# First batch of a two-scale attention kernel: q, k of later pairs loaded ahead of v, two q sums on POOL, and the last pair's transposes copied by two engines

## The reference

```
q_d, k_d, v_d = mean over each 4 positions of q, k, v          # 144 positions
out_up    = repeat(softmax(q_d k_d^T / 8) v_d, 4)              # coarse, full attention
out_local = softmax(q k^T / 8 where |i - j| < 4) v             # fine, a band
x = (out_up + out_local) laid out as 2304 tokens x 512
x = leaky_relu(x w_in1, 0.01) w_out1
h = x w_in2;  out = (h - tanh(h)) w_out2
```

## Time and profile before

| | |
|---|---|
| median of three runs | 960.9 us |
| the profiled execution | 960.35 us, of which span 958.6 us |
| PE busy | 942.1 us (98%) |
| PE weight loads busy | 884.8 us (92%) |
| DVE / ACT / POOL busy | 547.4 / 559.8 / 403.8 us |
| chain that ended last | PE 82%, POOL 6%, ACT 4%, issue 3%, DVE 2%, DMA 2% |
| granted clock in 40 slices | 8 tenths in the first slice, 9 or more tenths in every other |
| first slice (24 us) | PE 7 tenths busy, DVE 6, ACT 4, POOL 3, DMA 6 |

### The profile page before, as it was taken

How to read it: one execution, slowest core, us unless ns; L and a number is a source line. 1 busy time by engine, 2 the same in 40 slices (tenths; PEclk the granted TensorE clock), 3 DMA queues, 4 the chain that set the end, 5 groups by cost and what they waited for, 6 DMA issues and landing times.

```text
span 958.6 us, 19883 instructions
## 1 busy us (share of the span) xinstructions
PE 942.1 (98%) x6996; PEld 884.8 (92%) x6996; DVE 547.4 (57%) x1098; ACT 559.8 (58%) x1355; POOL 403.8 (42%) x343
## 2 busy tenths in 40 slices
PE   7999999999999999999999999999999999999998
PEld 6789999999999999999999999899899898898997
DVE  6754355435634543553235576776676766766764
ACT  4765546446445455454455677675666666656754
POOL 3584616427236246163342757433233232333232
PEclk8999999999999999999999999999999999999999
DMA  6875112211221121112002112000000000000000
GB/s 141 199 203 140 27 28 50 51 26 25 50 48 26 27 50 26 26 27 67 1 1 93 52 56 82 12 29 1 34 0 0 33 0 0 33 0 0 34 1 33
DMA packets 87797, 41.48 MB, mean 43 GB/s; under 512 B 60352, under 2 KB 81344, under 8 KB 87744
## 3 DMA queue, kind: packets, MB, share of 16 engines
q1 hardware_dynamic: 87744, 40.78, 16.3%
HBM read 36.04 MB, written 4.72 MB: 43 GB/s over the span
## 4 chain that ended last, share of the span: by engine, by line
PE 82%; POOL 6%; ACT 4%; issue 3%; DVE 2%; DMA 2%; SPq 1%; POOLq 0%; ACTq 0%; DVEq 0%
PE ph L520 13%; PE ph L521 12%; PE ph L522 12%; PE acc L596 6%; PE acc L549 6%; PE acc L597 6%; PE acc L598 6%; PE acc L550 6%; PE acc L551 6%; PE banks L418 2%; PE banks L450 2%; PE banks L437 2%; POOL g_lo L1135 1%; POOL in_lo L1114 1%; POOL w_lo_b L1142 1%
## 5 line engine op out<-in xcount | busy, mean ns | idle before, releaser
L1135 POOL TENSOR_TENSOR g_lo<-scratch,g_hi 128x384 fp32r<-128x384 f32 x96 | 126.1, 1313 | 257.1 <-ACT g_hi L723 257.1
L983 DVE TENSOR_TENSOR ph<-g,ph 128x288 f32<-128x288 f32 x128 | 59.0, 461 | 162.2 <-ACT g L737 161.7
L520 PE MATMUL ph<-x_hi,w_hi_a 128*128 128x288 f32 (+1 forms) x448 | 143.5, 320 | 0.8 <-DVE xT L873 0.5
L522 PE MATMUL ph<-x_hi,w_lo_a 128*128 128x288 f32 (+1 forms) x448 | 140.0, 312 | 0.0
L521 PE MATMUL ph<-x_lo,w_hi_a 128*128 128x288 f32 (+1 forms) x448 | 140.0, 312 | 0.0
L1114 POOL TENSOR_TENSOR in_lo<-w_whole,in_hi 128x512 fp32r<-128x512 f32 x64 | 82.5, 1290 | 130.9 <-ACT in_hi L703 130.9
L737 ACT ACTIVATE g<-ph 128x288 f32<-128x288 f32 x128 | 52.5, 410 | 130.8 <-PE ph L522 130.8
L1119 POOL TENSOR_TENSOR out_lo<-w_whole,out_hi 128x512 fp32r<-128x512 f32 x64 | 86.2, 1346 | 73.7 <-ACT out_hi L707 73.5
L1017 DVE SCALAR_TENSOR_TENSOR scratch<-scratch,ph 128x384 f32<-128x384 f32 x96 | 53.2, 554 | 110.1 <-ACT scratch L786 105.5
L785 ACT ACTIVATE scratch<-ph 128x384 f32<-128x384 f32 x96 | 46.7, 487 | 108.4 <-PE ph L522 106.8
L970 DVE TENSOR_TENSOR g_lo<-ph,g_hi 128x288 fp32r<-128x288 f32 x128 | 58.6, 458 | 59.1 <-ACT g_hi L723 59.1
(11 more groups left out here) (275 smaller groups left out, 2673.0 us busy)
## 6 DMA issues: line engine op xcount, KB each, us to landing
out_dram<-o_stage SPq DMA_DIRECT2D x18, 256.0 KB, 2.0
w_whole<-in_moe_w_in_dram SPq DMA_DIRECT2D x16, 256.0 KB, 3.9
w_whole<-in_moe_w_out_dram SPq DMA_DIRECT2D x16, 256.0 KB, 4.5
qn<-in_q_dram SPq DMA_DIRECT2D x26, 144.0 KB
kn<-in_k_dram SPq DMA_DIRECT2D x26, 144.0 KB
v4n<-in_v_dram SPq DMA_DIRECT2D x26, 144.0 KB
vw<-in_v_dram SPq DMA_DIRECT2D x26, 122.5 KB
scratch<-in_moe_w_in_dram SPq DMA_DIRECT2D x8, 256.0 KB, 2.8
```

The source lines that it names most:

```text
L520: pe.matmul(bank, whi, x_hi[:, c, 0:width], start=(c == 0), stop=False)
L522: last = pe.matmul(bank, wlo, x_hi[:, c, 0:width], start=False, stop=(c == CD - 1))
L983: dve.tensor_tensor(ph1[:, f % 2, 0:T1], g1[:, f % 2, :], ph1[:, f % 2, 0:T1], ALU.max)\
L1135: pool.tensor_tensor(g2_lo[:, f % 3, :], g2[:, f % 2, :], g2_hi[:, f % 3, :].bitcast(F32), ALU.subtract).then_inc(g_lo_done, 1)
```

## The change

The changed kernel differs in the first batch only.

1. SP issues the q, k loads of pair C ahead of pair A's v, and those of D4 ahead of B's v.
2. POOL makes the q sums of pairs C and D4: two adds of 128 x 144 with a stride of four on q, using `up` as scratch, then one add for each head (64 x 144) into `qd_diag`. DVE's step 3 is left out for these pairs. The sum stands at C's step 1 and D4's step 2 of POOL's program.
3. POOL's v sum moves from step 6 to step 11 for A and B and to step 10 for C; it stays at 6 for D4.
4. Of D4's four turned banks, DVE copies the two in bank 0 (steps 12, 14), which ACT did before.
5. C's last step (16) is moved to slot 26. On PE it is cut in two: blocks 0 to 3 come after D4's step 12, blocks 4 to 7 at slot 26, ahead of D4's step 15. The two fill matmuls after D4's step 14 go.
6. ACT splits kept weight block 0 at slot 23 instead of 24; ACT's and DVE's splits of x move to later slots, DVE's for parts 2 and 3 to the end.

```diff
-KEPT_SLOTS = (24, 27)
-FILL = {("a", 1): 2, ("a", 3): 2, ("b", 1): 1, ("b", 3): 2, ("c", 14): 3, ("d", 14): 2}
-X_HI_SLOTS = {23: (0, 1), 27: (2,)}
-X_LO_SLOTS = {24: (0, 1), 27: (2,)}
+KEPT_SLOTS = (23, 27)
+FILL = {("a", 1): 2, ("a", 3): 2, ("b", 1): 1, ("b", 3): 2, ("c", 14): 3}
+X_HI_SLOTS = {26: (0, 1), 28: (2,)}
+X_LO_SLOTS = {27: (0, 1)}
+LATE_C = (STEPS - 1, 26)
...
             load_qk(B, 0, 2)
+            load_qk(C, 0, 4)
             load_v(A, 0, 0)
-            load_qk(C, 0, 4)
+            load_qk(D4, 0, 6)
             load_v(B, 0, 2)
-            load_qk(D4, 0, 6)
             load_v(C, 0, 4)
...
+            def values_of_c(n0, n1):
+                for n in range(n0, n1):
+                    for h in range(2):
+                        last = pe.matmul(C.banks[h * D:(h + 1) * D, 0, n * QB:(n + 1) * QB], C.vw[:, n, h, :],
+                                         C.pT[:, slot_of(h, n), h * QB:(h + 1) * QB], start=True, stop=True)
+                return last
...
-                attention(step, s, i)
+                if s is C and step == LATE_C[0]:
+                    values_of_c(4, 8).then_inc(C.bank_full[0], 1)
+                else:
+                    attention(step, s, i)
+                if s is D4 and step == 12:
+                    values_of_c(0, 4)
...
+                elif step == 12 and s is D4:
+                    dve.wait_ge(s.bank_full[0], uses0(i, 5))
+                    dve.tensor_copy(s.pT[:, 4:8, :].rearrange("p n q -> p (n q)"), s.banks[0:WIN, 0, 0:4 * P])\
+                        .then_inc(s.bank_free[0], 1)
+                elif step == 14 and s is D4:
+                    dve.wait_ge(s.bank_full[0], uses0(i, 6))
+                    dve.tensor_copy(s.pdT[:, 1, :], s.banks[0:HALF, 0, 0:QT * QP]).then_inc(s.bank_free[0], 1)
...
+            def sum_q(s):
+
+                pool.wait_ge(zeros_set, 1)
+                pool.wait_ge(s.bank_free[1], uses1(0, 1))
+                pool.wait_ge(s.bank_free[0], uses0(0, 1))
+                q4 = s.qT[:, :].rearrange("p (t f) -> p t f", f=FACTOR)
+                pool.tensor_tensor(s.up[:, :], q4[:, :, 0], q4[:, :, 1], ALU.add).then_inc(s.q_summed, 1)
+                pool.wait_ge(s.q_summed, 1)
+                pool.tensor_tensor(s.up[:, :], s.up[:, :], q4[:, :, 2], ALU.add).then_inc(s.q_summed, 1)
+                pool.wait_ge(s.q_summed, 2)
+                for h, done in ((1, s.q_summed), (0, s.means_done)):
...
+            v_sum_step = {A: 11, B: 11, C: 10, D4: 6}
+
             def attention(step, s, i):
-                if step == (6 if first_of(i) else 5):
+                if (s is C and step == 1) or (s is D4 and step == 2):
+                    sum_q(s)
+                if step == (v_sum_step[s] if first_of(i) else 5):
```

More of the change, by code:

```diff
@@ L174, in __init__ @@
                 self.v_summed, self.vd_done = sem(f"v_summed_{which}"), sem(f"vd_done_{which}")
+                self.q_summed = sem(f"q_summed_{which}")
                 self.up_done = sem(f"up_done_{which}")
@@ L269, in batch0 @@
                 for at, s in sorted(places, key=lambda place: (place[0] % STEPS >= 6, -(place[0] % STEPS))):
-                    yield slot, at, s, 0
+                    if not (s is C and at == LATE_C[0]):
+                        yield slot, at, s, 0
+                if slot == LATE_C[1]:
+                    yield slot, LATE_C[0], C, 0
         def kept_at(slot):
@@ L671, in attention @@
                         .then_inc(s.bank_free[1], 1)
-                elif step == 12:
+                elif step == 12 and s is not D4:
                     act.wait_ge(s.bank_full[0], uses0(i, 5))
@@ L679, in attention @@
                     act.activation(s.pdT[:, 0, :], s.banks[0:HALF, 1, P:P + QT * QP], ACT.Copy).then_inc(s.bank_free[1], 1)
-                elif step == 14:
+                elif step == 14 and s is not D4:
                     act.wait_ge(s.bank_full[0], uses0(i, 6))
@@ L885, in attention @@
             def attention(step, s, i, batch, c):
-                if step == 3:
+                if step == 3 and s not in (C, D4):
                     dve.wait_ge(s.bank_free[1], uses1(i, 1))
@@ L1059, in _ @@
                 attention(step, s, i, i, FIRST.index(s))
-            lo_of_first_x(CD - 1)
+            for c in range(2, CD):
+                lo_of_first_x(c)
             mixed(0, nothing)
@@ L1082, in _ @@
         def _(pool):
+            def sum_q(s):
[8 more added lines that the diff above has]
+                for h, done in ((1, s.q_summed), (0, s.means_done)):
+                    rows = slice(h * D, (h + 1) * D)
+                    pool.tensor_tensor(s.qd_diag[rows, :, h, :], s.up[rows, :].rearrange("p (n m) -> p n m", n=NB),
+                                       q4[rows, :, 3].rearrange("p (n m) -> p n m", n=NB), ALU.add).then_inc(done, 1)
+                    if h:
+                        pool.wait_ge(s.q_summed, 3)
+            v_sum_step = {A: 11, B: 11, C: 10, D4: 6}
             def attention(step, s, i):
-                if step == (6 if first_of(i) else 5):
+                if (s is C and step == 1) or (s is D4 and step == 2):
+                    sum_q(s)
+                if step == (v_sum_step[s] if first_of(i) else 5):
                     pool.wait_ge(s.v_loaded, 128 * i + 128)
@@ L1095, in attention @@
                     ins.then_inc(s.vd_done, 1)
-                elif step == 9:
+                if step == 9:
                     pool.wait_ge(s.inv_l, i + 1)
```

## The result

The changed kernel takes 961.91 us (median of 18 executions), the kernel before 961.03 us (18 on the same chip): +0.88 us. The ratio of the two sets is 1.0025, 95% interval [1.0015, 1.0036], so the change makes the kernel slower; no change was forecast. The ratio says more than the medians because the changed kernel's times fall in two groups. Thirteen executions lie from 961.1 to 962.8 us, five from 963.9 to 968.4 us; all 18 of before lie from 959.9 to 961.8. The means differ by 2.26 us (963.26 against 961.00): some 0.8 us of it is in every execution, 1.4 us comes from the long ones. The thirteen short ones alone lie 0.82 us above the kernel before (an estimate by resampling the recorded times: 0.5 to 1.1 us), so that part is told from no change without the long ones. Both parts have to be explained.

A forecast was written before the change was run, and what follows sets the result against it. PE's own work bounds the kernel from 49.50 us on, so only the start of layer 1 counts: -0.1 + 1.4 - 0.6 = +0.7 us, set against the median of the runs, gives 961.6 us, range 958.5 to 963.1.

The forecast's parts named there:

- Step 1: Loads of the first batch: C's q DMAs go 4.41 us earlier, and both waits of PE for a DMA go.
- Step 2: POOL's q sum of C ahead of A's `pl`, a new wait for PE: -0.1 us, from -0.8 to +1.1.
- Step 3: PE's clock at C's scores: falls all the same, later; scores again take 2.99 us, timing unchanged (-0.1 us).
- Step 4: DVE without two q sums: worth nothing on the path; its wait for C's scores grows beyond 2.87 us.
- L: Start of PE's first layer matmul, where layer 1 begins, at 49.50 us before; forecast to move by +0.7 us.
- Step 5: C's v sum behind C's `pl` on POOL: PE waits at D's turn, +1.4 us, range +0.9 to +1.6.
- Step 6: End of first batch: -0.85 us from D's turn to L, x_lo about 0.3 us late; -0.6, range -0.9 to 0.
- Sum: The terms added at L: -0.1 + 1.4 - 0.6 = +0.7 us, giving 961.6 us.
- How the numbers follow: Chances for the whole kernel: faster 0.21, same 0.64, slower 0.15, with 0.2% (1.9 us) told from no change.
- the likeliest case: First batch: clock falls once and POOL is late at D; 961.6 us, own range 960.4 to 962.9, chance 0.50.
- the clock falls a second time: PE's 1.4 us wait at 42.7 us brings 1.2 GHz into layer 1: +2.7 on top of +0.7, 964.3 us; chance 0.10.
- the clock stays high: No fall before C's scores, which end at 23.0 instead of 24.83 us: -1.5 us in all, 959.4 us; chance 0.34.

The follow-up runs named there:

- the best version: Changed kernel with both q sums on DVE, C's v sum at step 8, POOL's ident and band earlier, eight start fills: 957.86 us, repeated 958.98 us.

## Why the prediction was wrong

Point by point, by its own steps:

- **Step 1** right: C's q at 14.79 us (14.8 said), no DMA wait.
- **Step 2** right: 20.87 us (20.75 said), the sum 2.36 us (2.2), its end at 19.62 (19.2). Of the two orders it left open, POOL went first. The nearness is in part luck: a sum 0.4 us later and the better order cancel.
- **Step 3** right for this execution: the clock falls later, and C's scores are at 21.87 us against 21.84.
- **Step 4** right in its price, but its sign did not come: DVE's wait for C's scores was to grow beyond 2.87 us and is 2.63, behind a subtraction held for 1.5 us; with the q sum given back, L lies 3.7 us earlier (46.28 against 50.01, with C's v sum moved too). DVE's sum costs nothing there, POOL's costs 1.5 us at A's `pl` and all that hangs on it.
- **Step 5** right: +1.34 us (44.03 - 42.67 less the 0.02 of step 2), +1.4 said. C's first v add took 1.31 us, held by DVE, where 0.72 is its price.
- **Step 6** right: -0.85 us from D's turn to L, as said, and x_lo of part 2 starts 0.35 us late behind L (0.3 said), which is 0.47 by the second block.
- **Sum**: +0.7 said; +0.98 in the trace once layer 1 runs, +0.88 in the medians. The time, 961.91 against 961.6, is within the range.

The step that failed is **How the numbers follow**: it said that a measurement can tell about 0.2%, 1.9 us, from no change, and so put the likeliest case, +0.7 us, wholly under "same". The term itself was sized rightly. With 18 executions of each kernel the 95% interval of the ratio reaches 1.0 to 1.1 us to either side, and the thirteen short executions alone, +0.82 us with some 0.3 to either side, are told from no change.

Under it lies a second fault, the assumption of steps 1 and 3 that there is one course of the clock. All terms were read off one execution, in which PE is at 2.4 GHz before A's scores. I took the two DMA waits that go for pure cost. They were slack as well: with the full clock forced to come after B's scores, the kernel before has its L at 49.55 us, and the changed kernel at 55.02, since its wait for POOL hangs on PE's own earlier work and moves along with it. About a third of its executions are long and give the mean another 1.4 us; both that were traced start in this way. I had this nowhere among the rivals. The nearest, *the clock falls a second time* (0.10), was traced once, with C's q sum on DVE and 1.49 us of waiting at 42.5 us; by their mean clock two of the 43 executions of the changed kernel probably had it too. Its price of +2.7 on top was too low: the low stretch lasted 20 us and not 5, and the execution took 8.3 us more than the one of 962.22 us with the same late start (an estimate, since that kernel differs in D's q sum and C's v sum). Behind a start at full clock, *the clock stays high* was traced in the best version alone, which has 1.27 us of waiting there; with twelve fills, six executions of the changed kernel fit it by their time and mean clock.

Shown: the cost of a late clock in either kernel, its picture in two long executions of the changed kernel, and the shorter end by itself (in its distances; its 0.3 us in the time are not told from nothing). The price of POOL's order at D is read from a run with two edits. Not settled: what decides, from one execution to the next, whether PE has its full clock before A's scores; fills from 1.54 us on did not. Nor is any of the eight long ones of before traced; by the mean clock one at most is of this kind.

One behaviour that steps 2, 5 and 6 used shows in both directions: DVE's subtraction takes 2.31 us for 0.82 where POOL is at work first, and POOL's v add 1.31 for 0.72 where DVE is. By the Trainium skill, page SBUF — State Buffer, section "SBUF: two separate sides", a DVE instruction with two SBUF inputs and a POOL instruction that reads SBUF exclude each other for the whole instruction, whichever is first; the trace agrees. DVE's TENSOR_SCALAR on 96x3, with one input, is held as well: 0.69 us at 37.35 while that v add runs, and 0.15 at 21.41 with POOL idle.

## What to carry to other kernels

A wait for a load has a fixed end, so it takes up whatever came late before it; a wait for another engine's answer to one's own work moves along with every delay. Before replacing the first by the second, ask what the time is when everything ahead runs 3 us later, and look at more than one execution. Work moved to an idle engine is free only if nothing that the bound engine waits for is queued behind it: here DVE's q sum cost nothing and POOL's cost 1.5 us. And before calling a small difference invisible, work out the interval from the spread and the number of executions.

## What the runs showed of the hardware

- The granted clock column reads 1.00 before the first recorded fall, also where matmuls run at 1.2 GHz: the execution of 968.59 us has a mean clock of 1.000 and three sets of scores at 2.99 us.
- The same kernel gets its full clock before A's scores in one execution and after C's in another. Fills from 2.54 us on (12 records, 2.93 us) are in all three traces of the changed kernel.
- An idle time of 1.07 us on PE at 48.5 to 49.6 us was followed by some 3.4 us at 0.50; one of 1.27 us at 18.0 to 19.3 us once was and once was not; one of 1.49 us at 41.0 to 42.5 us was followed by some 20 us.
- POOL's add of 144 elements with a stride of four took 0.45 and 0.56 us, two of 64 partitions 1.19 us. The line through the larger adds gives 0.41 us for 144 elements (an estimate), so the stride costs little, and half the partitions are no cheaper.
